# Eight steps of a complex running product through PSUM, two products moved from VectorE to GpSimd

## The reference, cut to what matters

```python
B, H, S, D = 2, 8, 768, 48
mag = np.sqrt(a_re * a_re + a_im * a_im)
scale = np.minimum(mag, 0.999) / (mag + 1e-06)
a_re_n, a_im_n = a_re * scale, a_im * scale
for t in range(S):
    ar, ai = a_re_n[:, :, t, :, None], a_im_n[:, :, t, :, None]
    new_re = ar * S_re - ai * S_im
    new_im = ar * S_im + ai * S_re
    kv = np.einsum('bhd,bhe->bhde', k[:, :, t], v[:, :, t])
    S_re, S_im = new_re + kv, new_im
    y[:, :, t] = np.einsum('bhd,bhde->bhe', q[:, :, t], S_re)
x = _moe_ref(y as 1536 rows of 384, w_gate, w1, w2, capacity)     # 8 experts, d_ff 1024
out = ((x @ w_a) * (x @ w_b)) @ w_out                             # d_ff 1536
```

## Time and profile before

| | |
|---|---|
| median of 3 executions | 578.49 us (577.61 to 579.61) |
| the profiled execution, its time | 578.43 us |
| its span, first to last instruction | 577.2 us |
| mean granted TensorE clock | 0.972 of full |
| busy | TensorE 534.1 us (93%), VectorE 372.6 (65%), ScalarE 296.3 (51%), GpSimd 51.0 (9%) |
| chain that ended last | TensorE 83%, VectorE 10%, ScalarE 5% |

### The profile page before, as it was taken

One profiled execution on the slowest core, in us unless ns is written; L12 is line 12 of the kernel. 1 busy time (PEld: TensorE's weight loads), 2 busy tenths in 40 slices (PEclk: granted clock), 3 DMA queues, 4 the chain that ended last, 5 costly groups with the idle time before them and its releaser, 6 DMA issues.

```text
span 577.2 us, 10681 instructions
## 1 busy us (share of the span) xinstructions
PE 534.1 (93%) x3951; PEld 486.9 (84%) x3952; DVE 372.6 (65%) x924; ACT 296.3 (51%) x705; POOL 51.0 (9%) x63
## 2 busy tenths in 40 slices
PE   0499697799999989999999999999999999999996
PEld 0276365599999989999999998888888888999996
DVE  5899999978888898988888876444321221222221
ACT  5666357765546577788777764433232121322322
POOL 1000000001121142000000000530020000200101
PEclk9877698999999999999999999999999999999999
DMA  8999022499323137656776649620010000100000
GB/s 319 283 386 352 4 102 72 156 252 319 85 70 82 42 110 232 244 194 217 258 259 206 229 121 70 160 83 0 1 55 1 0 1 0 57 1 1 28 0 28
DMA packets 46323, 73.31 MB, mean 127 GB/s; under 512 B 16520, under 2 KB 38792, under 8 KB 45384
## 3 DMA queue, kind: packets, MB, share of 16 engines
q1 hardware_dynamic: 44360, 67.97, 38.6%
q0 software_dynamic: 1920, 4.75, 2.6%
HBM read 55.76 MB, written 16.97 MB: 126 GB/s over the span
## 4 chain that ended last, share of the span: by engine, by line
PE 83%; DVE 10%; ACT 5%; issue 1%; DMA 1%; POOL 0%; DVEq 0%; POOLq 0%; ACTq 0%
PE psum L1392 26%; PE psum L1362 13%; PE psum L1129 11%; PE psum L1186 11%; PE psum L906 4%; PE psum L707 4%; PE psum L857 3%; PE psum L908 3%; PE psum L280 3%; PE psum L281 2%; DVE region L425 2%; DVE region L372 1%; PE psum L462 1%; DVE queries L425 1%; ACT region L308 1%; DVE region L377 1%
## 5 line engine op out<-in xcount | busy, mean ns | idle before, releaser
L1407 DVE TENSOR_TENSOR ga<-ga,psum 128x512 f32<-128x512 f32 (+1 forms) x48 | 26.6, 555 | 123.7 <-PE psum L1392 115.8
L1411 ACT ACTIVATE gh<-ga 128x512 fp32r<-128x512 f32 (+1 forms) x48 | 25.2, 525 | 82.1 <-DVE ga L1407 78.6
L1405 ACT ACTIVATE ga<-psum 128x512 f32<-128x512 f32 (+1 forms) x48 | 23.5, 491 | 73.8 <-PE psum L1392 66.8
L280 PE MATMUL psum<-region,ident 128*128 128x384 f32 (+1 forms) x42 | 25.9, 711 | 32.0 <-ACT region L290 22.6
L1129 PE MATMUL psum<-xh,w1h 128*128 128x224 f32 x192 | 52.7, 275 | 1.6 <-DVE xl L1012 1.6
L1186 PE MATMUL psum<-hh,w2h 128*128 128x224 f32 x192 | 53.9, 281 | 0.0
L1129 PE MATMUL psum<-xh,w1l 128*128 128x224 f32 x192 | 52.7, 274 | 0.0
L1129 PE MATMUL psum<-xl,w1h 128*128 128x224 f32 x192 | 52.7, 274 | 0.0
L1186 PE MATMUL psum<-hh,w2l 128*128 128x224 f32 x192 | 52.6, 274 | 0.0
L1186 PE MATMUL psum<-hl,w2h 128*128 128x224 f32 x192 | 52.6, 274 | 0.0
L1392 PE MATMUL psum<-yh,wah 128*128 128x512 f32 (+1 forms) x144 | 48.8, 339 | 0.0
(11 more groups left out here) (200 smaller groups left out, 1488.9 us busy)
## 6 DMA issues: line engine op xcount, KB each, us to landing
raw<-w SPq DMA_DIRECT2D x14, 1536.0 KB, 6.7
sorted_x<-region SPq DMA_DIRECT2D x8, 579.0 KB, 14.6
queries<-qk SPq DMA_DIRECT2D x4, 1152.0 KB, 25.5
xrow<-sorted_x SPq DMA_DIRECT2D x7, 579.0 KB, 6.9
region<-x_rows SPq DMA_DIRECT2D x14, 288.0 KB
queries<-w SPq DMA_DIRECT2D x2, 1536.0 KB, 15.3
x_rows<-region SPq DMA_DIRECT2D x5, 576.0 KB, 3.3
region<-a SPq DMA_DIRECT2D x2, 1152.0 KB, 8.7
```

Of the source, the lines that this page charges most:

```text
L280: nc.tensor.matmul(x, ident[:], x0[:, cut], start=True, stop=False)
L1405: m = act.done(ss.activation(x, ba[:, 0:w], ACT.Copy))
L1407: m = dve.done(tt(x, x, bb[:, 0:w], ALU.mult))
L1411: m = act.done(ss.activation(h_, x, ACT.Copy))
```

## The change

Steps 36 to 43 of the scan are made by a new function `scan_psum`. It keeps the running product in PSUM: banks 1 and 2 are a ring of two groups of two steps (`hist`), and of the partial products one half goes to PSUM bank 0 (`half`) and the other stays in `by`. A step has four multiplications of 96 elements and two additions of 96, where it had two of 192 and two of 96. `copy_steps` lets ScalarE copy two steps (384 elements) from the ring to the planes; the additions of a step wait for the copy of the step four before it, and VectorE waits for the last copy behind the scan. Two of quarter 1's products, ("x", 0) and ("q", 1), are made by GpSimd (`by_pool`), after step 36, and their turns are issued behind the copies of steps 38-39 and 40-41. The turns of quarters 0 and 1 use banks 6 and 7 alone; before they used 6, 7, 0, 1 and 2. The squares of steps 36 to 43 wait for the copies.

```diff
--- before.py
+++ after.py
@@ -377,6 +377,54 @@
                         m_step[i].append(dve.done(tt(walk(AT_Z[1] + now + k_ * D, [SA, 2], [1, D]),
                                                      by[k_][:, 0], by[k_][:, 1], ALU.add)))
 
+            RING, GS = 2, 2
+            m_copy, m_by = {}, {}
+
+            def hist(i, lo):
+
+                g_, r = divmod(i - lo, GS)
+                return bank[1 + g_ % RING][:, 0:2 * GS * PAIR].rearrange("p (u i k d) -> p u i k d", u=2, i=GS, d=D)[:, :, r]
+
+            def half(k_):
+                return bank[0][:, k_ * PAIR:(k_ + 1) * PAIR].rearrange("p (v d) -> p v d", v=2)
+
+            def scan_psum(i, lo):
+
+                now, prev = i * PAIR, (i - 1) * PAIR
+                m = []
+                for n_, (p0, p1) in enumerate(PIECES):
+                    if p0 <= i < p1:
+                        dve.wait(m_neg[n_], m_sra[n_])
+                if i == lo:
+                    for b in range(1 + RING):
+                        dve.wait(*(free[b] or ()))
+                    dve.wait(*m_read[0])
+                for k_ in range(2):
+                    dve.wait(m_step[i - 1][k_])
+                    for u in range(2):
+                        if i == lo:
+                            x = walk(AT_Z[2 - u] + prev + k_ * D, [0, 2], [1, D])
+                        else:
+                            x = hist(i - 1, lo)[:, 1 - u, k_].unsqueeze(1).broadcast_to([P, 2, D])
+                        m.append(dve.done(tt((by[k_][:, 0], half(k_))[u], x,
+                                             walk(AT_Z[u] + now + k_ * D, [SA, 2], [1, D]), ALU.mult)))
+                m_by[i], m_step[i] = m[-1], []
+                for k_ in range(2):
+                    dve.wait(m[2 * k_], m[2 * k_ + 1])
+                    if i - RING * GS in m_copy:
+                        dve.wait(m_copy[i - RING * GS])
+                    m_step[i].append(dve.done(tt(hist(i, lo)[:, :, k_], by[k_][:, 0], half(k_), ALU.add)))
+
+            def copy_steps(i, lo):
+
+                last = i + GS - 1
+                act.wait(*m_step[last], *([m_by[last + 1]] if last + 1 in m_by else []))
+                m = act.done(ss.activation(walk(AT_Z[1] + i * PAIR, [SA, 2], [1, GS * PAIR]),
+                                           bank[1 + (i - lo) // GS % RING][:, 0:2 * GS * PAIR].rearrange(
+                                               "p (u w) -> p u w", u=2), ACT.Copy))
+                for j in range(i, i + GS):
+                    m_copy[j] = m
+
             SETS = [1, 0, 1, 0]
             B_AT = [AT_X + 4 * BLK, AT_Q + 4 * BLK, AT_V, AT_Z[0]]
             assert P // 2 * D >= 2 * W
@@ -391,7 +439,8 @@
                 return flat(B_AT[s] + i * W, W)
 
             def slot_squares(s, lo=0, hi=3):
-                act.wait(m_step[TI * s + TI // 3 * hi - 1][1])
+                i = TI * s + TI // 3 * hi - 1
+                act.wait(m_copy.get(i, m_step[i][1]))
                 if s == 3:
                     act.wait(m_turn[3 * TI // TB - 1])
                     ss.wait_ge(s_xrows[0], 32)
@@ -409,27 +458,28 @@
                 act.wait(m)
                 m_le[s] = act.done(ss.activation(B_(s, 1)[:, cut], B_(s, 0)[:, cut], ACT.Exp, scale=-1.0))
 
-            def product(s, x, n, cuts=1):
-
-                vv.wait_ge(s_qk[s], 16)
+            def product(s, x, n, cuts=1, by_pool=False):
+
+                q_ = pool if by_pool else dve
+                q_.e.wait_ge(s_qk[s], 16)
                 if s:
-                    dve.wait(*(m_prod[s - 1, *y] for y in PLACES))
+                    q_.wait(*(m_prod[s - 1, *y] for y in PLACES))
                 if (x == "x") == (n == 1):
-                    dve.wait(m_kx[s])
+                    q_.wait(m_kx[s])
                 k_at = AT_KQ + s * 2 * W + (0 if (x == "x") == (n == 1) else W) + n * D
                 m_cut[s, x, n] = []
                 for u in range(cuts):
                     w = TI // cuts
                     i0 = u * w if n else TI - (u + 1) * w
                     o = DST[s][x, n] + 2 * D * (i0 if n else TI - 1 - i0)
-                    m = dve.done(tt(walk(o, [1, 2], [2 * D if n else -2 * D, w], [2, D]),
-                                    walk(AT_Z[1] + s * W + n * D + i0 * PAIR, [SA, 2], [PAIR, w], [1, D]),
-                                    walk(k_at + i0 * PAIR, [0, 2], [PAIR, w], [1, D]), ALU.mult))
+                    m = q_.done(q_.e.tensor_tensor(walk(o, [1, 2], [2 * D if n else -2 * D, w], [2, D]),
+                                                   walk(AT_Z[1] + s * W + n * D + i0 * PAIR, [SA, 2], [PAIR, w], [1, D]),
+                                                   walk(k_at + i0 * PAIR, [0, 2], [PAIR, w], [1, D]), ALU.mult))
                     m_cut[s, x, n].append(m)
                 m_prod[s, x, n] = m
                 if x == "x":
                     beta = SL + s if n else SL - 1 - s
-                    sp.wait_ge(dve.sem, m[1])
+                    sp.wait_ge(q_.sem, m[1])
                     sp.dma_start(x_rows[:, beta * TI:(beta + 1) * TI, :],
                                  flat(DST[s][x, n], W).rearrange("p (t c) -> p t c", c=C2)).then_inc(s_xrows[s], 16)
 
@@ -559,11 +609,25 @@
                 ss.wait_ge(s_vw[b], 16)
             for x, n in (PLACES[3], *PLACES[:3]):
                 product(0, x, n)
-                turn(0, x, n, (6, 7, 0, 1, 2))
-            for x, n in PLACES:
+                turn(0, x, n, (6, 7))
+            for x, n in (("x", 1), ("q", 0)):
                 product(1, x, n)
-                turn(1, x, n, (6, 7, 0, 1, 2))
-            scan(3 * TI, 4 * TI - 4)
+                turn(1, x, n, (6, 7))
+            S0, S1 = 3 * TI, 4 * TI - 4
+            scan_psum(S0, S0)
+            pool.wait(m_step[S0][1])
+            for x, n in (("x", 0), ("q", 1)):
+                product(1, x, n, by_pool=True)
+            for i in range(S0, S1, GS):
+                for j in range(max(i, S0 + 1), i + GS):
+                    scan_psum(j, S0)
+                    if j == i and i > S0:
+                        copy_steps(i - GS, S0)
+                if i >= S0 + 4:
+                    turn(1, *(("x", 0), ("q", 1))[(i - S0 - 4) // 2], (6, 7))
+            copy_steps(S1 - GS, S0)
+            free[0] = free[1] = free[2] = [m_step[S1 - 1][1], m_copy[S1 - 1]]
+            dve.wait(m_copy[S1 - 1])
             slot_squares(3, 0, 2)
             slot_sum(3, 0, 2)
             inverse_times(2)
```

## The result

The changed kernel takes 584.94 us (median of 5 executions, 582.81 the lowest) against 578.58 for the kernel before; the ratio is 1.0095, with a 95% interval from 1.0055 to 1.0135, so 3.2 to 7.8 us slower. 584.3 was forecast. Ratios and intervals in this document leave out executions whose clock was lower over the whole kernel (here one of the five, 606.03 us at a granted clock of 0.94, where the others have 0.965 to 0.979), so a ratio can differ from the quotient of its two medians.

A forecast was written before the change was run, and what follows sets the result against it. VectorE's chain before 113 us bounds the kernel, and ScalarE's queue there has no spare time. VectorE's shift of +5.8 us on 578.43 gives 584.2, said as 584.3 with the median's 0.06; range 583 to 586, with rivals 581.0 to 588.0.

The forecast's parts named there:

- The bound and the place: Around 87 to 115 us: VectorE carries the chain up to 113 us; a microsecond more there is one at the end.
- ScalarE's queue order: Step copies stand behind 18 to 24 turns in ScalarE's in-order queue; VectorE goes on at 101.6 instead of 95.80, +5.8 us.
- the ring's wait: Additions of step 40 wait for copy 36-37, as the ring holds four steps; VectorE idle nearly 6 us.
- the last copy's wait: The first VectorE instruction behind the scan waits for copy 42-43: from 100.1 to 101.6 us.
- The bank cycle: Turns on two banks: one bank's cycle is 1.315 us for two turns, 0.66 a turn against 0.485.
- rival 1: Two banks do not slow the turns, 0.487 us each: only +2.7 us, 581.2 us; chance 0.10.
- The new step: Scan steps 36 to 43 on VectorE: six 96-element instructions, 1.02 us instead of 0.875, +1.16 us over eight steps.
- GpSimd's products: Two products moved off VectorE, -2.54 us there; 1.27 to 4.6 us each on GpSimd, hidden, costed at nothing.
- the bound above of 4.6: Upper limit in us for one GpSimd product, scaled whole from 382 ns for 96 elements to 1152 elements.
- Rival 3: ScalarE is not in the way and VectorE's saving shows, resuming 0.8 us earlier: 577.6 us; chance 0.05.
- Rival 2: Granted clock falls to half during the turns, bank cycle 1.74 us: +10.4 us, 588.8 us; chance 0.08.
- Rival 4: VectorE's change stands elsewhere, for example a late inverse of the last quarter at low clock: +7 to +9 us, 587; chance 0.05.

The follow-up runs named there:

- e7: Changed kernel with three of the four step copies moved ahead in ScalarE's queue, all 24 turns still before the last copy: 584.59 us, ratio 1.0101.
- e8: Kernel of e7 with VectorE's wait for the last step copy moved from ahead of the squares to ahead of step 44: 582.32 us, ratio 1.0067.
- e5: Changed kernel with early step copies, last copy and squares ahead of ten turns, those on five banks, later VectorE wait, two warm calls dropped: 579.46 us, ratio 1.0012.
- e6: Kernel of e3 with the two GpSimd products back on VectorE: 581.62 us, ratio 1.0037.
- e2: Changed kernel with the two GpSimd products back on VectorE, after step 36: 584.85 us, ratio 1.0110.
- e3: Changed kernel with bank 0's partial products kept in SBUF and that bank given to quarter 0 and 1 turns (6, 7, 0): 583.88 us, ratio 1.0087.
- e4: Kernel before with only the two products moved to GpSimd behind step 36, plain scan, turns on five banks: 585.32 us, ratio 1.0114.
- r3: Kernel of e5 profiled again, unchanged: 42.73 us from first product to first scores matmul, span 577.1 us.

## Why the prediction was right

- **The bound and the place.** VectorE before 113 us was the chain, and what was added there came out at the end: 6.2 us in the stage of the profile, 3.2 to 7.8 over the executions.
- **ScalarE's queue order** was the step that carried the forecast. The halt before the additions of step 40 was forecast at nearly 6 us and measured at 5.89; the second at about 1.5 us and measured at 1.43. e7 adds that the first halt was a symptom: without it the time is the same. The text named the ring's wait and the last copy's wait without saying which of them decides. It is the second, and with it the squares' place behind the same turns: moving the wait alone gave 2.4 us (e8), and only e5, which also takes the squares forward, got below the kernel before.
- **The bank cycle** was worked out at 1.315 us from single readings and is 1.34. Behind the first turn, copy 36-37 was forecast at 11.49 us and came at 11.74, and VectorE went on at 17.29 instead of 16.92: this is the difference between the forecast 5.8 and the stage's 6.2. The price of the missing bank was shown by e6 against e2: 3.36 us, where the forecast implied 3.1 (5.8 less the 2.7 of rival 1).
- **The new step**: 1.02 forecast by the addition's row, 1.03 measured. The rule of the Trainium skill on VectorE with PSUM (VectorE: DVE Perf Modes, the section on the TRN2 errata), from which 65 ns an instruction had been estimated, does not show: the multiplications that write SBUF have a mean of 249 ns with one input in PSUM and of 250 with both in SBUF (step 36), and those that write PSUM have 256. The row was the better guide.
- **GpSimd's products**: 2.6 us each; the bound above of 4.6, scaled from an instruction of 96 elements, was far off: from 96 to 1152 elements the time grew from 0.38 to 2.61 us, 2.1 ns an element, so about 0.18 of that instruction's 0.38 do not grow with the size (an estimate from two instructions of different shape). The 2.6 cycles an element of the Trainium skill (GPSIMD Engine Reference, section 3.1), estimated at 2.5 us, agree with the trace. Costing the products at nothing held (e2). The text did not see that they can run beside the scan only because the steps read PSUM; e3 and e4 show the price without that.
- **The rivals.** Rival 1 (no loss by two banks) is refuted by the pairs in the trace. Rival 3 (VectorE's own saving shows) is what e5 makes of nearly the same work, 1.3 us in two of three profiles' stages, by taking ScalarE out of the way. Rival 2 (clock falls in the turns) did not happen in the changed kernel's profile, where it was 1.00 from 86 to 106, but did in e4, e8 and r3. Rival 4 did not happen: VectorE did not wait before the last inverse, which came 6.18 us later, as the one before it. The prediction says that its range reaches most of the way to this rival; the rival's price, +7 to +9, lies inside 581.0 to 588.0 altogether.
- **How near it came**: 584.3 against 584.94 is closer than the method is, and that much of it is luck. The stage was forecast 0.4 us short, and four of the five executions of the changed kernel lie between 582.8 and 589.1.

## What to carry to other kernels

Before giving work to an engine "with 51% busy", look at its queue in the stretch itself and write down what stands in it ahead of the thing that others will wait for; a copy that becomes part of the critical chain inherits everything issued before it. When buffers are taken away from a pipeline of two engines, work out the cycle of one buffer (fill, handover, drain, handover) and divide by their number: here a cycle of 1.34 us and a drain of 0.49 need three banks. And if a halt has been removed and the time stays, follow the same queue to its next reader.

## What the runs showed of the hardware

- VectorE instructions with two SBUF inputs and GpSimd's `tensor_tensor` exclude each other: 0.45 us of additions took 4.91 beside GpSimd's products (e3), and 5.22 us of products took 12.23 beside a gapless scan (e4). With one VectorE input in PSUM neither was slower: 5.22 us of products beside steps of 1.03 us, which is also a step without GpSimd (e2).
- The experts' first 72 matmuls took 8.3, 9.9 or 11.2 to 11.4 us in executions of either kernel, with granted clocks of 1.00, 0.86 and 0.73 over the 12 us from their start; steps of about 1.5 us in a kernel of 580 are as large as what such a change is worth, and only a stretch between two events shows it.
- TensorE and ScalarE passing PSUM banks to each other: with two banks two turns took 1.34 us, with three or five one followed another in 0.49 (e3).
